# Attention and two MLP layers on one core: averages of v and low parts of x on GpSimd in the first pairs, a block's first scores one place later

## The reference

```
# attention, batch 4, 8 heads, 576 positions, head 64
q_d, k_d, v_d = mean over groups of 4 positions          # 144 positions
out_d  = softmax(scale * q_d @ k_d.T) @ v_d
out_up = repeat each row of out_d 4 times
local  = softmax(scale * q @ k.T, only where |i - j| < 4) @ v
x = (out_up + local), as 2304 tokens x 512
# first MLP (512 -> 1536 -> 512)
g = x @ w_gate;  x = (silu(g) * (x @ w_val)) @ w_out
# second MLP (512 -> 2048 -> 512)
h = x @ w_in;    out = (max(h, 0) + alpha * min(h, 0)) @ w_out
```

## Time and profile before

| | us |
|---|---|
| median of 3 runs | 984.84 (984.21 to 985.62) |
| profiled execution | 983.52 |
| its span, first to last instruction | 981.7 |
| TensorE busy | 952.8 |
| VectorE busy | 549.7 |
| ScalarE busy | 247.0 |
| GpSimd busy | 134.1 |
| mean granted clock of TensorE | 0.997 of full |

### The profile page before, as it was taken

How to read it: one execution, slowest core, us unless ns; L and a number is a source line. 1 busy time by engine, 2 the same in 40 slices (tenths; PEclk the granted TensorE clock), 3 DMA queues, 4 the chain that set the end, 5 groups by cost and what they waited for, 6 DMA issues and landing times.

```text
span 981.7 us, 20376 instructions
## 1 busy us (share of the span) xinstructions
PE 952.8 (97%) x7912; PEld 889.7 (91%) x7912; DVE 549.7 (56%) x1171; ACT 247.0 (25%) x631; POOL 134.1 (14%) x151
## 2 busy tenths in 40 slices
PE   5899999899998999999999999999999999999998
PEld 3799999799997999999999999999999999999997
DVE  8777666566665666666564554444444444444443
ACT  3444222222221322222223541111111111111111
POOL 5576010010100101000013850000000000000000
PEclk9999999999999999999999999999999999999999
DMA  8465221221211211312105530010010100100000
GB/s 257 138 189 160 81 70 49 66 68 48 85 57 41 92 49 40 102 58 76 48 13 174 163 119 2 1 65 1 0 64 0 43 21 0 64 0 0 32 0 33
DMA packets 31735, 63.07 MB, mean 64 GB/s; under 512 B 2992, under 2 KB 14256, under 8 KB 31664
## 3 DMA queue, kind: packets, MB, share of 16 engines
q1 hardware_dynamic: 31664, 62.02, 20.0%
HBM read 52.57 MB, written 9.44 MB: 63 GB/s over the span
## 4 chain that ended last, share of the span: by engine, by line
PE 90%; DVE 3%; DMA 2%; issue 2%; POOL 2%; ACT 1%; SPq 0%; DVEq 0%; ACTq 0%; POOLq 0%
PE ps L975 50%; PE ps L1012 20%; PE ps L995 14%; PE ps L930 2%; DMA w_raw<-w 2%; PE ps L878 1%; POOL w_lo L428 1%; PE ps L886 1%; PE ps L938 1%; PE ps L916 1%; DMA qk<-qk 0%; DVE h_lo L806 0%; DVE qk_d_early L646 0%; DVE turned_alone L712 0%; DVE turned_one L712 0%
## 5 line engine op out<-in xcount | busy, mean ns | idle before, releaser
L975 PE MATMUL ps<-x_hi,w_hi 128*128 128x288 f32 x768 | 234.3, 305 | 0.7 <-DVE gated L816 0.2
L975 PE MATMUL ps<-x_lo,w_hi 128*128 128x288 f32 x768 | 228.7, 298 | 0.0
L975 PE MATMUL ps<-x_hi,w_lo 128*128 128x288 f32 x768 | 227.6, 296 | 0.0
L552 ACT CAST h_hi<-hidden 128x288 fp32r<-128x288 f32 (+1 forms) x192 | 90.9, 473 | 405.6 <-DVE hidden L843 332.0
L806 DVE TENSOR_TENSOR h_lo<-hidden,h_hi 128x288 fp32r<-128x288 f32 (+1 forms) x192 | 112.2, 585 | 70.0 <-ACT h_hi L552 66.8
L975 PEld LDWEIGHTS ps<-x_hi,w_hi 128*128 128x128 f32 x768 | 146.0, 190 | 4.8 <-issue 1.1
L841 DVE TENSOR_SCALAR gated<-ps,alpha_sb 128x384 f32<-128x384 f32 x96 | 59.3, 617 | 159.5 <-PE ps L975 159.5
L975 PEld LDWEIGHTS ps<-x_hi,w_lo 128*128 128x128 f32 x768 | 146.4, 191 | 0.0
L975 PEld LDWEIGHTS ps<-x_lo,w_hi 128*128 128x128 f32 x768 | 146.4, 191 | 0.0
L995 PE MATMUL ps<-h_hi,w_hi 128*128 128x288 f32 x384 | 115.6, 301 | 0.1
L1012 PE MATMUL ps<-w_lo,h_hi 128*128 128x512 f32 x288 | 113.2, 393 | 0.0
(11 more groups left out here) (123 smaller groups left out, 1423.1 us busy)
## 6 DMA issues: line engine op xcount, KB each, us to landing
w_raw<-w SPq DMA_DIRECT2D x68, 256.0 KB, 2.7
qk<-qk SPq DMA_DIRECT2D x30, 436.0 KB, 3.5
vsrc_one<-vsrc SPq DMA_DIRECT2D x29, 288.0 KB
vwin<-vwin SPq DMA_DIRECT2D x30, 192.0 KB, 2.3
y_t<-y_sb SPq DMA_DIRECT2D x8, 576.0 KB, 3.4
x_raw<-y_t SPq DMA_DIRECT2D x6, 768.0 KB, 5.6
out<-y_sb SPq DMA_DIRECT2D x5, 768.0 KB, 4.1
qk_early<-qk SPq DMA_DIRECT2D x2, 436.0 KB, 6.1
```

The source lines that it names most:

```text
L552: nc.scalar.copy(h_hi[r][:, 0:width], hidden[r][:, 0:width]).then_inc(h_hi_ready, 1)
L975: mm = nc.tensor.matmul(out_ps, w[:, piece, 128 * k:128 * k + 128], x_parts[low][:, k, :], start=(k == 0 and n == 0), stop=(k == KC - 1 an ...
```

## The change

GpSimd takes average_v of pairs 2 and 3 of block 0 as two additions each (first the halves of each group of four, then the two sums), and x_lo of pairs 0 to 2 of block 0. VectorE's order in the start is rewritten: average_v of pair 0 stands behind the reciprocals of pair 3, average_qk of block 1 behind the last x_lo, and the counts of `v_averaged` and `x_lo_ready` that GpSimd's work leaves open are added by hand. TensorE waits for the new semaphores `v_averaged_pool` and, ahead of the first block, `x_lo_early`. In all blocks the scores of pair 0 go from place 0 to place 1, their maxima and exponentials with them, and the reciprocals of pair 0 from place 2 to place 3. The other pairs keep their places.

```diff
--- before.py
+++ after.py
@@ -58,12 +58,18 @@
 POOL_PIECES = 2
 EARLY_PIECES = 6
 EARLY_HI = 14
+POOL_AVERAGES = 2
 BANK = 512
 STEPS1 = NB * C1
 TB2 = 384
 NB2 = TOKENS // TB2
 ALL = NB + NB2
 TT = TB2 // 128
+
+
+def scored_at(k):
+
+    return 0 if k else 1
 
 
 def act_pieces(k):
@@ -218,6 +224,9 @@
         vsrc_in = [sem(f"vsrc_in{r}") for r in range(PAIRS)]
         qk_averaged = sem("qk_averaged")
         v_averaged = sem("v_averaged")
+        v_halved = sem("v_halved")
+        v_averaged_pool = sem("v_averaged_pool")
+        x_lo_early = sem("x_lo_early")
         turned_zeroed = sem("turned_zeroed")
         scores_ready = sem("scores_ready")
         masked = sem("masked")
@@ -452,10 +461,28 @@
 
             for j in range(POOL_PIECES):
                 split_piece(j)
-            for k in range(PAIRS):
-                normalise(k, k, 0)
-            for j in range(POOL_PIECES, EARLY_PIECES):
-                split_rest(j)
+            def average_v(k):
+
+                pool.wait_ge(vsrc_in[k], 16)
+                v = vsrc_sb[0][k]
+                nc.gpsimd.tensor_tensor(v[:, :, :, 0:2], v[:, :, :, 0:2], v[:, :, :, 2:4], ALU.add).then_inc(v_halved, 1)
+                pool.wait_ge(v_halved, k - POOL_AVERAGES + 1)
+                nc.gpsimd.tensor_tensor(v_d[0][k][:, :, :], v[:, :, :, 0], v[:, :, :, 1], ALU.add).then_inc(v_averaged_pool, 1)
+
+            def split_x_lo(k):
+                pool.wait_ge(x_hi_ready, k + 1)
+                nc.gpsimd.tensor_tensor(x_lo[0][:, k, :], x_f32[0][k][:, :], x_hi[0][:, k, :].bitcast(F32), ALU.subtract).then_inc(x_lo_early, 1)
+
+            normalise(0, 0, 0)
+            normalise(1, 1, 0)
+            average_v(2)
+            normalise(2, 2, 0)
+            normalise(3, 3, 0)
+            average_v(3)
+            split_rest(2)
+            for k in range(PAIRS - 1):
+                split_x_lo(k)
+                split_rest(3 + k)
             for k in range(PAIRS):
                 first, end = act_pieces(k), act_pieces(k + 1)
                 for j in range(first, min(first + 2, end)):
@@ -554,7 +581,7 @@
             def attention(a, half, p):
 
                 k, at = divmod(p, SLOT)
-                if at == 1:
+                if at == scored_at(k) + 1:
                     local_exponentials(a, k, 1)
                     down_exponentials(a, k, 1)
                 if at == 5:
@@ -716,6 +743,8 @@
                 q = PAIRS * a + k
                 dve.wait_ge(att_ready, q + 1)
                 o = att_ps(mode, k)
+                if not mode and k:
+                    dve.wait_ge(x_added, k)
                 nc.vector.tensor_scalar(up[:, :], o[:, DOWN_O:DOWN_O + HQ], 1.0 / FACTOR, None, ALU.mult).then_inc(up_ready, 1)
                 dve.wait_ge(up_ready, q + 1)
                 nc.vector.tensor_tensor(x_f32[mode][k][:, :].rearrange("p (s f) -> p s f", f=FACTOR), o[:, 0:TB].rearrange("p (s f) -> p s f", f=FACTOR),
@@ -756,23 +785,20 @@
             local_maxima(0, 3, 0, 0)
             down_maxima(0, 3, 0)
             reciprocals(0, 2, 0)
-            average_v(0, 0)
             turn_local(0, 1, 0)
             reciprocals(0, 3, 0)
+            average_v(0, 0)
+            turn_local(0, 2, 0)
             average_v(0, 1)
             add_up(0, 0, 0)
-            turn_local(0, 2, 0)
-            average_v(0, 2)
-            split_x_lo(0, 0, 0, 0)
+            turn_local(0, 3, 0)
             add_up(0, 1, 0)
-            turn_local(0, 3, 0)
-            average_v(0, 3)
-            split_x_lo(1, 0, 1, 0)
             add_up(0, 2, 0)
-            average_qk(1, 0)
-            split_x_lo(2, 0, 2, 0)
             add_up(0, 3, 0)
             split_x_lo(3, 0, 3, 0)
+            average_qk(1, 0)
+            dve.sem_inc(v_averaged, PAIRS - POOL_AVERAGES)
+            dve.sem_inc(x_lo_ready, PAIRS - 1)
             dve.wait_ge(consts_ready, 2)
             dve.sem_inc(y13_copied, 4)
             dve.sem_inc(gated_ready, 1)
@@ -781,10 +807,10 @@
             def attention(a, half, p, next_too):
 
                 k, at = divmod(p, SLOT)
-                if at == 0:
+                if at == scored_at(k):
                     local_maxima(a, k, half, 1)
                     down_maxima(a, k, 1)
-                if at == 2:
+                if at == scored_at(k) + 2:
                     reciprocals(a, k, 1)
                 if at == 3:
                     average_v(a, k)
@@ -930,7 +956,10 @@
                         nc.tensor.matmul(o[rows, t * TQ:(t + 1) * TQ].rearrange("p (i q) -> p i q", q=GQ), vwin_sb[mode][k][:, t, rows],
                                          turned[mode][k][:, e * TILES + t, :, 0:GQ], start=True, stop=True)
                 pe.wait_ge(down_copied, q + 1)
-                pe.wait_ge(v_averaged, q + 1)
+                if mode or k < POOL_AVERAGES:
+                    pe.wait_ge(v_averaged, q + 1)
+                else:
+                    pe.wait_ge(v_averaged_pool, k - POOL_AVERAGES + 1)
                 for c in range(2):
                     for e in range(2):
                         rows = slice(HEAD * e, HEAD * e + HEAD)
@@ -965,6 +994,7 @@
                     pair_outputs(a, k, 1)
 
             pe.sem_inc(h_used, 2)
+            pe.wait_ge(x_lo_early, PAIRS - 1)
 
             PARTS = ((w_hi, 0), (w_hi, 1), (w_lo, 0))
```

## The result

| | us |
|---|---|
| before, median of 4 runs beside the changed kernel | 984.6 |
| changed kernel, median of 4 runs | 978.2 (977.2 to 979.45) |
| ratio | 0.9935, 95% interval 0.992 to 0.995 |
| profiled execution, its span | 977.23, 975.2 |

The account below looks back on a forecast made before the run. TensorE was taken as the bound, with 90% of the chain. Edges -5.6, blocks 1 to 6 +0.6, first block +0.9 and start +0.3 sum to -3.8 us: 984.84 becomes 981.0, range 978.4 to 985.6.

Parts of the forecast that it names:

- the edges: The loop's back edge on TensorE, passed twice: shorter code wait and clock kept up save 2.8 us each, together -5.6.
- blocks 1 to 6: Later reciprocals of pair 0 make TensorE's transposes wait 0.1 us for GpSimd's normalise in each block: +0.6 in all.
- the first block: Block 0: row_sum goes from 40.91 to 41.9, with w_lo of piece 8 and every later load behind it: +0.9 us.
- the second rest: TensorE's second idle stretch at each back edge, waiting for code: shrinks from 2.33 to 0.86 us, 1.5 saved.
- The clock's part: At each edge the granted clock stays at 1.00, so the next 24 products take 3.43 and not 4.72: 1.3 us saved.
- 2.0 us of cover are gone: Blocks 1 to 6: normalise, which ended 2.0 us before TensorE's transposes, now ends at 113.31, releasing them 0.1 late.
- the rival of a late normalise: Blocks from 1 on: h_lo takes 1.31, normalise ends 0.9 later, costing 6.0 instead of 0.6: 986.8; chance 0.07.
- The start: Up to TensorE's first product: TensorE resumes at 33.4 against 33.28 (+0.1), plus +0.2 for the port: +0.3 us.
- the clock stays up after an edge: Denies the rival that the clock falls anyway behind the back edges, price 2 x 1.3: 983.6; chance 0.22.
- the code wait is not counted from running out: Denies the rival that both edges keep 2.33 and the clock falls, leaving only costs: 986.6; chance 0.08.
- The losing start: Rival: GpSimd's adds at twice the time hold up w_lo, x_lo 2 and reciprocals, +2.2 instead of +0.3: 982.9; chance 0.12.
- start and first block gain: Rival: v lands earlier and earlier pieces leave slack, -0.5 and 0 instead of 0.3 and 0.9: 979.3; chance 0.14.

Follow-up runs that it names:

- number 9: Changed kernel plus 36 tiny matmuls on TensorE in the start's idle time, shifting the code behind them: 978.29 us.
- number 1: Kernel before with only the scores of pair 0, their maxima, exponentials and reciprocals one place later, old start kept: 978.52 us.
- number 3: Kernel before with, on TensorE alone, the first product group ahead of the scores inside place 0; other engines keep their places: 979.6 us.
- number 5: The changed kernel measured once more, nothing edited: 978.67 us.
- number 6: Changed kernel with the reciprocals of pair 0 back at place 2: 978.85 us.
- number 7: Changed kernel with VectorE's average of v of pair 0 ahead of the transposes of pair 1: 978.32 us.
- number 8: Changed kernel with average of v of pair 0 ahead of the transposes of pair 1 and reciprocals of pair 0 at place 2: 976.65 us.
- number 2: Changed kernel with all scores back at place 0, so only the start is rearranged: 986.27 us.
- number 4: Kernel before plus 36 tiny matmuls on TensorE in the start's idle time, shifting the code behind them, order kept: 979.22 us.
- number 11: Changed kernel with the three iterations of the first layer's loop written out on TensorE alone, without its If: 972.91 us.
- number 10: Changed kernel with the scores of pair 0 one place later still (place 2, reciprocals at 4): 991.39 us.

## Why the prediction was right or wrong

The direction, the place and the mechanism of the gain were right: faster, at the two edges, by a rest that work covers and a clock that stays up. The forecast gain was too small by 2.6 us, and three terms of the sum make it up: the edges 0.9, blocks 1 to 6 0.9 and the first block 0.8. The step that failed is their size, and most of all the second rest, put at 0.86 and measured at 0.33 and 0.05. The stated range also has a slip: by the terms of the sum, a gaining start with the code wait gone gives 984.84 - 7.3 + 0.6 - 0.5 = 977.6 and not 978.4, and the clock falling with all costs at their upper ends gives 987.4 and not 985.6.

**The edges, -5.6 forecast, -6.5 measured.** The clock's part was right: what is left of an edge without its rests is 3.05 - 1.79 = 1.26 and 3.47 - 2.33 = 1.14, where I had 1.3. The reason given for it is not shown: the clock stayed at all 16 edges of the unshifted kernels with this order, but in number 9 it fell once behind a single rest of 1.90. The term that was mis-sized is the second rest: 0.86 forecast, 0.33 and 0.05 measured, and 0.05 to 0.62 in numbers 1, 3 and 5 to 8, which have this order and unshifted code. I took the work in front as 2.2 us and it is 2.43, since the first group behind a rest takes 1.82 and not 1.6. And I took the code as coming 3.06 after the first instruction; it came after 2.76 and 2.48, and in number 6 after 3.04 (rests of 0.62 and 0.60). So that time varies by 0.6 from case to case. With the scores ahead it was 2.92 to 3.06 at four edges (kernel before and number 2), and I took it for an order in which it was mostly shorter. From the second packet of code to the work behind it stand 2.2 to 2.6 in all of these; what varies is the packet's own start behind the first matmul, 0.72 and 0.85 in the kernel before, 0.17 and 0.24 in the changed one, 0.79 and 0.67 in number 6. What sets that start is open. The first rests (1.54 and 1.49 before, 1.75 and 1.43 after) vary by chance (numbers 5 and 7). Both rests of both edges together are 4.1 shorter, where I had 2.9; with 0.2 less for the clock that is about the 0.9.
Numbers 4 and 11 and the packets say what kind of thing the rests are: the second goes when the code is shifted, both go with the jump, and each has a packet of code ahead of it. By the Trainium skill (Runtime: NRT & Kernel Launch, Instruction fetch mechanics) a taken branch has to wait for the block of its target when this lies outside the blocks at hand; the trace agrees, with first rests of 1.43 to 1.75 in the changed kernel and none in straight code.

**Blocks 1 to 6, +0.6 forecast, -0.3 measured** (0.15 and 0.18 of the marks). The step "2.0 us of cover are gone" was right to 0.2, but I let it go over by 0.1: normalise ends 0.17 ahead of the transposes at 113.59, and they have no wait. The small gain is a term that the sum left out. From the mark behind the first edge to the last one ahead of the second (117.98 before) numbers 1 and 3 have 0.18 and 0.17 less too, numbers 2 and 4 at most 0.02: it goes with the product group ahead of the scores. Number 10 shows how near the limit is: one place more costs 1.7 a block. The rival of a late normalise is out: h_lo takes 0.40 to 0.46 in block 1, not 1.31.

**The first block, +0.9 forecast, about +0.1 measured.** Its first half was right: row_sum went from 40.91 to 41.68 (forecast 41.9), and w_lo behind it from 42.99 to 43.64. The step that all later loads carry it unchanged failed. At the last piece of weights 0.45 was left (96.19 to 96.64) and at block 1 0.31, start included. From that last piece on, block 1 moves with it: +0.45 and +0.31 in the changed kernel, +1.93 and +2.02 in number 1, -0.54 and -0.71 in number 7. Between piece 8 and piece 35 the delay of the profiles changes by -1.3 to +1.0 (number 9: +0.25 to -1.00; number 5: +0.99 to +0.42; number 6: +0.68 to +1.65), so the loads pass it on only roughly. What takes it up was not settled.

**The start, +0.3 forecast, +0.25 measured** (33.53 against 33.28). "Nearly all turns into waiting" was right: TensorE's down product at 22.07 behind the average (forecast 22.35), VectorE with waits of 1.00, 0.79 and 0.78 for TensorE. GpSimd's first add came at 18.76 (forecast 18.3), the adds were a little shorter than taken, and the port hit was another one than I had named. GpSimd's timeline:

```profile
18.76 1.04 POOL L468 TENSOR_TENSOR vsrc_early<-vsrc_early 72x512 f32<-72x512 f32 x1 [2.47 <-DMA vsrc_early<-vsrc]
19.88 0.63 POOL L470 TENSOR_TENSOR v_d_early<-vsrc_early 72x256 f32<-72x256 f32 x1
...
32.07 0.79 POOL L474 TENSOR_TENSOR x_lo<-x_f_early,x_hi 128x288 fp32r<-128x288 f32 x1
```

1.04 + 0.63 are 1.67 a pair, against 1.9 taken and 3.8 kept as a bound. On VectorE the last x_lo met GpSimd's own:

```profile
32.32 0.85 DVE L755 TENSOR_TENSOR x_lo<-x_f_early,x_hi 128x288 fp32r<-128x288 f32 x1 [0.50 <-ACT x_hi L529]
```

0.85 where it was 0.46: 0.39 us on the path. By the Trainium skill (GPSIMD Engine Reference, Performance pitfalls for Q7 kernels) the second add would have cost 50% more for its stride; the measurement decides against it here: 0.63 for 72x256, beside 0.66 for 72x288 without such a stride.
I had also costed the new start against the old one, with the moved scores beside it. The profiles of numbers 1 and 2 show that this sum can't be split: each half alone costs 2.0 up to block 1. The +0.3 was right for the pair only.

Two more rivals are out: the clock stays up after an edge, and the code wait is not counted from running out, as its packet starts 0.17 and 0.24 us into 2.43 of work. The losing start is out too, at +0.25. Of the rival "start and first block gain" half came true, the part of the first block.

## What to carry to other kernels

Where a chain shows "issue" on the engine that is the bound, look for a jump just ahead of it, count the instructions up to the next rest, and put the longest work ahead of it; or write the loop out for that engine alone, which was worth 5.3 us more here for one edit. A time read from one kind of row (3.06 after the first instruction) is no constant until a second kind of row has it. A step that is moved away from the head of a queue changes what the queue's head waits for: cost the orders of all engines together. And measure the parts alone: here one part (number 1) has the whole gain in time, and the other alone loses.

## What the runs showed that I had not expected

- The rests of a back edge vary from profile to profile, of one kernel too (second rest 0.33 and 0.05 at the same edge): the first 1.43 to 1.97 us without the shifted code, 1.90 to 2.24 with it.
- The granted clock is not told by the length of a rest. It fell after 1.90 (number 9), 2.03 and 2.24 (number 4); it stayed after 1.92 (number 3), 1.99 (number 9, its second edge) and 1.97 (number 10). What decides is open.
- In the start the windows show a clock of 1.00 while products stand 0.24 us apart, twice their later distance of 0.13 (a window of the kernel before, three matmuls in 0.25 us):

```profile
37.00:37.25 0.25, 0.25 (x3) 0.25 (x2) 0.00 (x0) 0.00 (x0) 0.00 (x0) 1.00 0.69 270
```

  The trace has no record of the clock that early: its first one starts at 39.69 in this kernel, just where the products become quick (39.72), so the 1.00 ahead of it is not a measurement. By that first record TensorE became quick between 34.8 (number 7) and 39.9 (number 2), and at 36.8 and 39.4 in two executions of the changed kernel. The forecast took this pace as given.
- A first product group behind a rest takes 1.82 us at full clock, and 1.60 without a rest (number 11).
